# Experts of a fused attention, mixture-of-experts and channel-mix kernel: 256 tokens at a time with the first weights stationary

## The chip, the cores and the metric

The kernel runs on one core of one Trainium2 chip. A core has five engines with their own instruction streams: PE (TensorE, matrix products), DVE (VectorE), ACT (ScalarE), POOL (GpSimd) and SP (SyncE, here used for DMA alone). They share an on-chip memory (SBUF, 128 partitions) and eight banks that receive TensorE's results (PSUM, 128 partitions by 512 floats each). The metric is the device time of one execution in microseconds (us), the median of several runs. A profiled execution gives besides a trace of every instruction.

## The reference, cut to what matters

Three layers follow one another on 1536 tokens (2 sequences of 768) of width D = 512: a decayed linear attention, a mixture of 8 experts of which each token takes one, and a channel mix. The change concerns the second.

```python
for s in range(S):                      # per sequence
    fresh_e = int(np.argmax(logits[b, s]))
    if s == 0 or local_gate[b, s] < 0.5:
        e = fresh_e
    else:
        e = prev_e if prev_e >= 0 else fresh_e
    prev_e = e
    ...                                 # p: softmax of the token's logits
    h = np.maximum(x[b, s] @ w1[e], 0.0)        # w1[e]: 512 x 1024
    out[b, s] = p[e] * (h @ w2[e])              # w2[e]: 1024 x 512
```

## The kernel before

**Attention stage.** Twelve chunks of 128 tokens are computed in a software pipeline; each ends as x (128 tokens by 512), which is stored to `x_dram`, and as 9 logits a token.

**Dispatch.** From the logits each token's expert, and its place among the expert's tokens, are worked out on DVE with a few small products on PE: `rank`, `row` (place modulo 128) and `col` (expert and tile). Twelve one-hot matrices `slot_row` (POOL, L408) and twelve `slot_col` (DVE, L758) are multiplied on PE (L1017) into `slots`: for each tile of each expert the token numbers of its 128 rows. `plan` holds, for each expert, where its tiles start: an expert has as many tiles of 128 as its tokens fill, but at least `MIN_TILES = 2`. POOL gathers the rows of x for a tile by an indirect DMA (L433, L417) and scatters the result (L427).

**Experts.** For each expert a loop over its tiles. `tile` of the PE program (L1057) does: `h_products`, x times w1, with the tile's transposed x (128 columns) as the stationary operand and 512 columns of w1 moving, so that h comes out with tokens on partitions; ACT applies the ReLU into `h_sb` (L500); `h_transposes` (L1048) turns h on PE by blocks of 128x128 into `psT`; ACT copies that to `hh` (L505); `y_products` takes hh as the stationary operand and 512 columns of w2 moving; DVE copies y out of PSUM (L805). The next tile's x is transposed on PE in between (L1034).

**Three products.** Precision is held by splitting each float operand in two parts, high and low: ACT rounds a copy to the reduced format (`hh`, `xh`, `wh`), DVE subtracts it from the original (`hl` L784, `xl` L780, `wl` L790), and `three_products` multiplies high by high, high by low and low by high: three matmuls for each block (L1024 to L1026), each with its own weight load.

**Weights.** An expert's weights are 8 chunks (`CH`) of 128x1024: 4 of w1, 4 of w2. SP loads a chunk into `raw` (one buffer for the 8) when DVE has split the former content (`part_l`), two experts ahead; ACT and DVE split into one of two sets of `parts`, used by turns. This conversion for the next expert lies inside the first tile of an expert on both engines (`tile(i, e, p)`). PE waits at an expert's start for all eight chunks.

**Order.** It is written out by hand, engine by engine, with semaphores between them. `keep_warm` (L918) is idle work of PE on the identity matrix.

**After the experts.** The results come back from `y_dram` into `keep`, are weighted, transposed (L1104) and mixed; the channel mix runs in four blocks of 384 tokens. There w_k's 128x128 blocks are the stationary operand, and 384 columns of transposed tokens move.

## Time and profile before

| | us |
|---|---|
| median of 3 runs | 489.41 (488.84 to 490.62) |
| the profiled execution, its own time | 488.76 |
| its span from the first to the last instruction | 486.9 |
| PE busy | 459.2 |
| DVE busy | 260.4 |
| ACT busy | 210.9 |
| POOL busy | 92.6 |
| chunks of expert weights loaded in the loop (512 KB each) | 64 |

The time of a run contains some 2 us around the span. A matmul's duration runs from its start until its result has been written; several are under way at once, so what one costs on PE is the distance between the starts of two, not its duration. PEld is the weight load of a matmul, which the trace shows apart. A line number is that of the code above; a buffer's number is left out of its name (`bank` is any of the eight PSUM banks).

### The profile page before, as it was taken

The page shows a single profiled execution, that of the slowest core. Times are in us where ns is not written, and L with a number is a line of the kernel's source. Part 1 is how long each engine was busy: PE and PEld are TensorE (multiplying, and loading weights), DVE is VectorE, ACT ScalarE, POOL GpSimd, SP SyncE. Part 2 cuts the span into 40 slices and gives each one's busy share as a digit, 9 for nine tenths or more (in the row PEclk, how much of TensorE's full clock was granted, in tenths as well). Part 3 has the DMA queues.
Part 4 walks back from the last instruction along what each step waited for, and adds up shares of the span by engine and source line. Part 5 has one row for each costly group of instructions (what it writes and reads, how often), then busy time and mean ns, then how long its engine had stood idle before and what let it go on. Part 6 is the DMA issues. An engine that isn't in the chain of part 4 may idle for free.

```text
span 486.9 us, 7685 instructions
## 1 busy us (share of the span) xinstructions
PE 459.2 (94%) x2635; PEld 391.4 (80%) x2636; DVE 260.4 (53%) x421; ACT 210.9 (43%) x337; POOL 92.6 (19%) x137
## 2 busy tenths in 40 slices
PE   7899997699999999999999996599999999999997
PEld 7788886577878787878788884498899889889985
DVE  2677885355564737473829194495444544616401
ACT  1133331073645545464636373487244533714400
POOL 2436752522221222222222221000000000000000
PEclk9899999799999999999999999599999999999999
DMA  6999881048392929393867500700010000010001
GB/s 218 406 398 329 327 313 66 22 139 299 113 311 99 309 96 296 115 284 144 261 256 239 192 29 27 268 1 0 22 46 0 22 22 22 0 43 22 0 23 43
DMA packets 28460, 70.87 MB, mean 146 GB/s; under 512 B 3154, under 2 KB 4178, under 8 KB 28436
## 3 DMA queue, kind: packets, MB, share of 16 engines
q1 hardware_dynamic: 22946, 57.95, 33.8%
q0 software_dynamic: 2800, 9.18, 5.7%
q10 hardware_dynamic: 2690, 3.44, 2.0%
q8 instruction: 14, 0.23, 0.2%
q14 instruction: 10, 0.08, 0.1%
HBM read 59.53 MB, written 11.02 MB: 145 GB/s over the span
## 4 chain that ended last, share of the span: by engine, by line
PE 80%; DVE 9%; issue 3%; DMA 3%; POOL 2%; DVEq 1%; ACT 0%; SPq 0%; POOLq 0%; ACTq 0%
PE bank L1024 21%; PE bank L1026 20%; PE bank L1025 20%; DVE wl L790 5%; PE bank L954 3%; PE bank L943 2%; PE bank L930 2%; PE bank L964 2%; PE bank L1048 2%; PE bank L972 2%; PE bank L1034 2%; POOL slot_row L408 1%; PE bank L918 1%; PE bank L979 1%; DVE hl L784 1%
## 5 line engine op out<-in xcount | busy, mean ns | idle before, releaser
L790 DVE TENSOR_TENSOR wl<-raw,wh 128x1024 fp32r<-128x1024 f32 x64 | 74.6, 1218 | 0.0
L509 ACT ACTIVATE wh<-raw 128x1024 fp32r<-128x1024 f32 x64 | 64.1, 1054 | 0.0
L784 DVE TENSOR_TENSOR hl<-bank,hh 128x512 fp32r<-128x512 f32 x32 | 22.1, 690 | 64.0 <-ACT hh L505 64.0
L1024 PE MATMUL bank<-wh,hh 128*128 128x512 f32 x128 | 52.8, 412 | 2.6 <-DVE hl L784 1.6
L1024 PE MATMUL bank<-wh,xh 128*128 128x512 f32 x128 | 51.4, 402 | 1.7 <-DVE xl L780 1.7
L1026 PE MATMUL bank<-wh,hl 128*128 128x512 f32 x128 | 50.2, 392 | 0.0
L1026 PE MATMUL bank<-wh,xl 128*128 128x512 f32 x128 | 50.0, 391 | 0.0
L1025 PE MATMUL bank<-wl,hh 128*128 128x512 f32 x128 | 49.8, 389 | 0.0
L1025 PE MATMUL bank<-wl,xh 128*128 128x512 f32 x128 | 49.8, 389 | 0.0
L500 ACT ACTIVATE h_sb<-bank 128x512 f32<-128x512 f32 x32 | 19.1, 596 | 64.8 <-PE bank L1026 64.8
L1024 PE MATMUL bank<-xkh,wh 128*128 128x384 f32 x128 | 43.0, 336 | 0.3 <-DVE xkl L856 0.3
L1026 PE MATMUL bank<-xkh,wl 128*128 128x384 f32 x128 | 42.8, 334 | 0.0
L1025 PE MATMUL bank<-xkl,wh 128*128 128x384 f32 x128 | 42.8, 334 | 0.0
L1024 PE MATMUL bank<-wh,kkh 128*128 128x512 f32 x96 | 37.4, 389 | 0.0
L1025 PE MATMUL bank<-wl,kkh 128*128 128x512 f32 x96 | 37.4, 389 | 0.0
L1026 PE MATMUL bank<-wh,kkl 128*128 128x512 f32 x96 | 37.4, 389 | 0.0
L1024 PEld LDWEIGHTS bank<-wh,hh 128*128 128x128 f32 x128 | 24.0, 188 | 12.9 <-issue 9.1
L864 DVE TENSOR_TENSOR kk<-kk 128x384 f32<-128x384 f32 x32 | 17.7, 557 | 31.2 <-ACT kk L587 31.2
L505 ACT ACTIVATE hh<-bank 128x512 fp32r<-128x512 f32 x32 | 19.1, 597 | 29.7 <-PE bank L1048 29.7
L874 DVE TENSOR_TENSOR o_sb<-bank,r_sb 128x512 f32<-128x512 f32 x12 | 8.3, 690 | 41.6 <-PE bank L1026 41.6
L587 ACT ACTIVATE kk<-bank 128x384 f32<-128x384 f32 x32 | 15.5, 490 | 34.5 <-PE bank L1026 34.5
L1024 PEld LDWEIGHTS bank<-wh,xh 128*128 128x128 f32 x128 | 24.1, 188 | 6.2 <-issue 1.9
(159 smaller groups left out, 894.2 us busy)
## 6 DMA issues: line engine op xcount, KB each, us to landing
raw<-in_w_dram SPq DMA_DIRECT2D x64, 512.0 KB, 8.0
qk_sb<-in_qk_dram SPq DMA_DIRECT2D x12, 512.0 KB, 7.0
kv_sb<-in_kv_dram SPq DMA_DIRECT2D x12, 512.0 KB, 6.1
x_dram<-keep ACTq DMA_DIRECT2D x12, 256.0 KB, 6.2
keep<-y_dram SPq DMA_DIRECT2D x12, 256.0 KB, 5.3
out_dram<-o_sb SPq DMA_DIRECT2D x12, 256.0 KB, 2.0
raw<-in_w_k_dram SPq DMA_DIRECT2D x4, 512.0 KB
raw<-in_w_v_dram SPq DMA_DIRECT2D x4, 512.0 KB
```

The lines of the kernel that those rows point to most:

```text
L500: act.activation(h_sb[:, g * D:(g + 1) * D], bank[g][:, :], ACT.Relu).then_inc(s["h_done"], 1)
L505: act.activation(hh[:, 4 * g:4 * g + 4, :], by(psT[g][:, :], 4), ACT.Copy).then_inc(s["hh_done"], 1)
L509: act.activation(parts[1 - p][0][:, c, :], raw[:, c, :], ACT.Copy).then_inc(s["part_h"], 1)
L587: act.activation(kk[f % KK], bank[f % 4][:, 0:HB], ACT.Relu).then_inc(s["relu_done"], 1)
L784: dve.tensor_tensor(hl[:, 4 * g:4 * g + 4, :], by(psT[g][:, :], 4), hh[:, 4 * g:4 * g + 4, :].bitcast(F32), ALU.subtract).then_inc(s["hl_d ...
L790: dve.tensor_tensor(parts[1 - p][1][:, c, :], raw[:, c, :], parts[1 - p][0][:, c, :].bitcast(F32), ALU.subtract).then_inc(s["part_l"], 1)
L864: dve.tensor_tensor(kk[f % KK], kk[f % KK], kk[f % KK], ALU.mult).then_inc(s["kk_done"], 1)
L930: mm = pe.matmul(psS[t % 2][a][:, pair * P:(pair + 1) * P], lhsT=kT[r, pair, :], rhs=qT[r, pair, :], start=True, stop=True)
L954: mm = pe.matmul(psO[DH * a:DH * (a + 1), pair * P:(pair + 1) * P], lhsT=kv_sb[t % RING][:, 1, h * DH:(h + 1) * DH], rhs=AT[t % 2][:, a, p ...
L1024: pe.matmul(ps, lhsT=a_high, rhs=b_high, start=start, stop=False)
L1025: pe.matmul(ps, lhsT=a_high, rhs=b_low, start=False, stop=False)
L1026: return pe.matmul(ps, lhsT=a_low, rhs=b_high, start=False, stop=stop)
```

## The change

The unit of work of an expert becomes 256 tokens (`PAIR`), two gathered tiles side by side. The first product is turned round: 128 columns of w1 are the stationary operand and the 256 tokens of the unit move, so h comes out transposed, with the hidden dimension on partitions, four PSUM banks with two blocks of 128x256 each. ACT applies the ReLU straight from PSUM into `hh`, DVE makes `hl` from the same bank, and `h_sb` with its transposes is gone. The second product is as before, once for each half of the unit. An expert has at least one unit. The 8 chunks of weights are split in two groups: the first six are converted before the unit, the last two (`CH_LATE`) behind it, and PE waits for the first six ahead of the first product and for all eight ahead of the second. In the dispatch, DVE makes the one-hot matrices in two operations of each kind (128x576 and 128x768) instead of twelve, POOL multiplies one of them by the token numbers, and a short chain on DVE works out the column of `slots` with which each unit starts (`unit_col`).

```diff
-    MIN_TILES = 2
-    NTILES_MAX = N // P + MIN_TILES * E
+    PAIR = 2 * P
+    UNITS_MAX = N // PAIR + E
+    CH_LATE = 2
     CH = KD + KF // 2
     FIRST = 1
+    PARTS = FIRST + CH_LATE
...
 @block.gpsimd
-            pool.wait_ge(s["row_done"], 1)
-            for n in range(NT):
-                pool.tensor_scalar(slot_row[:, n, :], iota_row[:, :], row[:, n:n + 1], None, ALU.is_equal).then_inc(s["slot_row_done"], 1)
+            pool.wait_ge(s["value_done"], 1)
+            for b in range(B):
+                pool.wait_ge(s["col_hit_done"], b + 1)
+                pool.tensor_tensor(slot_col[:, b * NC:(b + 1) * NC, :], col_hit[:, b * NC:(b + 1) * NC, :], per_token(value, b),
+                                   ALU.mult).then_inc(s["slot_col_done"], 1)
+            def fetch(rows):
+                for a in range(2):
+                    pool.indirect_dma_start(out=x_tok[a], out_offset=None, in_=x_dram[:, :],
+                                            in_offset=bass.IndirectOffsetOnAxis(ap=rows[:, a:a + 1], axis=0)).then_inc(x_in[a], 16)
...
+                pool.wait_ge(s["x_ps_done"], u * 2 + 2)
+                pool.tensor_copy(x_slots[:, :], slots[:, bass.ds(next_c, 2)]).then_inc(s["x_slots_done"], 1)
...
+                fetch(x_slots)
+                for a in range(2):
+                    pool.wait_ge(s["y_done"], u * 2 + FIRST + a + 1)
...
+                    pool.indirect_dma_start(out=y_dram[:, :], out_offset=bass.IndirectOffsetOnAxis(ap=y_slots[:, a:a + 1], axis=0),
+                                            in_=y_sb[a], in_offset=None).then_inc(y_out[a], 16)
...
 @block.scalar
-            def relu_h(i, g):
-                act.wait_ge(s["h_ps"], i * 2 + g + 1)
-                act.activation(h_sb[:, g * D:(g + 1) * D], bank[g][:, :], ACT.Relu).then_inc(s["h_done"], 1)
+            def h_high(u, f):
+                act.wait_ge(s["h_ps"], u * 4 + f + 1)
+                act.activation(hh[:, 2 * f:2 * f + 2, :], by(psH[f][:, :], 2), ACT.Relu).then_inc(s["hh_done"], 1)
+            def unit(u):
+                for f in range(4):
+                    h_high(u, f)
+                for a in range(2):
+                    x_high(u + 1, a)
...
-                    tile(lo, e, p)
+                    act.wait_ge(s["raw_in"], (e + 1) * (16 * (CH - CH_LATE)))
+                    act.sem_inc(s["act_passed"], 1)
+                    for c in range(CH - CH_LATE):
+                        if c == KD:
+                            act.wait_ge(s["y_ps"], lo * 2 + FIRST)
+                            act.sem_inc(s["act_passed"], 1)
+                        weights_high(p, c)
...
+                    with act.Fori(lo, hi) as u:
+                        unit(u)
+                    act.wait_ge(s["raw_late"], (e + 1) * (16 * CH_LATE))
+                    act.sem_inc(s["act_passed"], 1)
+                    for c in range(CH - CH_LATE, CH):
+                        weights_high(p, c)
...
 @block.vector
-            for n in range(NT):
-                dve.tensor_scalar(slot_col[:, n, :], iota_row[:, 0:COLS], col[:, n:n + 1], value[:, n:n + 1],
-                                  ALU.is_equal, ALU.mult).then_inc(s["slot_col_done"], 1)
+            for b in range(B):
+                dve.tensor_tensor(col_hit[:, b * NC:(b + 1) * NC, :], iota_row[:, 0:COLS].unsqueeze(1).to_broadcast([P, NC, COLS]),
+                                  col[:, b * NC:(b + 1) * NC].unsqueeze(2).to_broadcast([P, NC, COLS]), ALU.is_equal).then_inc(s["col_hit_done"], 1)
+                dve.tensor_tensor(slot_row[:, b * NC:(b + 1) * NC, :], iota_row[:, :].unsqueeze(1).to_broadcast([P, NC, P]),
+                                  row[:, b * NC:(b + 1) * NC].unsqueeze(2).to_broadcast([P, NC, P]), ALU.is_equal).then_inc(s["slot_row_done"], 1)
...
+            def h_low(u, f):
+                dve.wait_ge(s["hh_done"], u * 4 + f + 1)
+                dve.scalar_tensor_tensor(out=hl[:, 2 * f:2 * f + 2, :], in0=by(psH[f][:, :], 2), scalar=0.0,
+                                         in1=hh[:, 2 * f:2 * f + 2, :].bitcast(F32), op0=ALU.max, op1=ALU.subtract).then_inc(s["hl_done"], 1)
+            def y_copy(u, a):
+                dve.wait_ge(s["y_ps"], u * 2 + FIRST + a + 1)
+                dve.wait_ge(y_out[a], u * 16 + 16)
+                dve.tensor_copy(y_sb[a], psY[a][:, :]).then_inc(s["y_done"], 1)
+            def unit(u):
+                for f in range(4):
+                    h_low(u, f)
+                y_copy(u, 0)
+                for a in range(2):
+                    x_low(u + 1, a)
+                y_copy(u, 1)
...
-                    tile(lo, ep * UNROLL + j, p)
+                    for c in range(CH - CH_LATE):
+                        weights_low(e, p, c)
...
+                    with dve.Fori(lo, hi) as u:
+                        unit(u)
+                    for c in range(CH - CH_LATE, CH):
+                        weights_low(e, p, c)
...
 @block.tensor
-            def h_transposes(i, g):
...
+            def h_products(p, f):
+                for i in range(2):
+                    cols = slice((2 * f + i) * P, (2 * f + i + 1) * P)
+                    for c in range(KD):
+                        mm = three_products(psH[f][:, i * PAIR:(i + 1) * PAIR], [w[:, c, cols] for w in w1p[p]],
+                                            [x[:, c, :] for x in (xh, xl)], start=(c == 0), stop=(c == KD - 1))
+                mm.then_inc(s["h_ps"], 1)
+            def y_products(u, p, a):
+                for f in range(KF):
+                    if a == 0 and f % 2 == 0:
+                        pe.wait_ge(s["hl_done"], u * 4 + f // 2 + 1)
+                    mm = three_products(psY[a][:, :], [x[:, f, a * P:(a + 1) * P] for x in (hh, hl)], [w[:, f, :] for w in w2p[p]],
+                                        start=(f == 0), stop=(f == KF - 1))
+                mm.then_inc(s["y_ps"], 1)
+            def unit(u, e, p):
+                pe.wait_ge(s["xl_done"], u * 2 + 2)
+                for f in range(4):
+                    h_products(p, f)
+                pe.wait_ge(s["part_l"], e * CH + PARTS)
+                pe.wait_ge(s["y_done"], u * 2 + FIRST)
+                y_products(u, p, 0)
+                x_unit_transposes(u + 1)
+                y_products(u, p, 1)
...
-                    pe.wait_ge(s["part_l"], FIRST + e * CH)
+                    pe.wait_ge(s["part_l"], e * CH + PARTS - CH_LATE)
```

What this does to the order of instructions on PE, in an expert's work: this is a tile of before, from the last products of the first three quarters of h to the first products of y. `wh_49` and `wl_50` are the high and low parts of the weights, the last figure is rows by moving columns, and rows of one product that repeat are left out.

```order
L1026 MATMUL bank<-wh_49,xl 128x512
L1046 REGISTER_ALU
L1048 MATMUL bank<-ident,h_sb 128x128 x4
L1024 MATMUL bank<-wh_49,xh 128x512
...
L1024 MATMUL bank<-wh_49,hh 128x512
L1025 MATMUL bank<-wl_50,hh 128x512
...
L1046 REGISTER_ALU
L1048 MATMUL bank<-ident,h_sb 128x128 x4
L1030 ISA
L1034 MATMUL bank<-ident,x_tok 128x128 x4
L1024 MATMUL bank<-wh_49,hh 128x512
```

And this is a unit of the changed kernel, from the end of h to the second half of y, on the same engine; its products of h are 96 with 256 columns where two tiles of before had 48 with 512.

```order
L1038 MATMUL bank<-xh,wl_50 128x256
L1071 REGISTER_ALU
L1072 REGISTER_ALU
L1062 ISA
L1036 MATMUL bank<-wh_49,hh 128x512
L1037 MATMUL bank<-wl_50,hh 128x512
...
L1043 ISA
L1045 REGISTER_ALU
L1047 MATMUL bank<-ident,x_tok_79 128x128 x4
L1047 MATMUL bank<-ident,x_tok_80 128x128 x4
L1036 MATMUL bank<-wh_49,hh 128x512
```

The transposes of `h_sb` are gone, and those of x for the next unit stand together between the two halves of y.

On DVE an expert of before begins with the split of its first h, and the conversion of the next expert's weights (`wl`) lies between the steps of the first tile:

```order
L784 TENSOR_TENSOR hl<-bank,hh 128x512
L789 ISA
L790 TENSOR_TENSOR wl_52<-raw,wh_51 128x1024
...
L784 TENSOR_TENSOR hl<-bank,hh 128x512
L779 REGISTER_ALU
L780 TENSOR_TENSOR xl<-bank,xh 128x512
...
L804 ISA
L805 COPY y_sb<-bank 128x512
```

In the changed kernel the copy of the second half of y is followed by the two late chunks of one set and the six early ones of the other (each row of `wl_50` stands for one of six), and only then by the split of h:

```order
L799 COPY y_sb_82<-bank 128x512
...
L804 TENSOR_TENSOR wl_52<-raw,wh_51 128x1024
L803 REGISTER_ALU
L804 TENSOR_TENSOR wl_52<-raw,wh_51 128x1024
L803 ISA
L804 TENSOR_TENSOR wl_50<-raw,wh_49 128x1024
...
L830 ISA
L793 SCALAR_TENSOR_TENSOR hl<-bank,hh 128x512
```

So eight conversions in a row now stand between a unit's last copy and the next unit's first `hl`.

## Rows read from the trace of the kernel before

**Rows 1.** The page, shares of the chain that ended last, by engine.

```profile
PE 80%; DVE 9%; issue 3%; DMA 3%; POOL 2%; DVEq 1%; ACT 0%; SPq 0%; POOLq 0%; ACTq 0%
```

**Rows 2.** Groups by form: count, busy us, mean ns, idle before and its releaser.

```profile
L784 DVE TENSOR_TENSOR hl<-bank,hh 128x512 fp32r<-128x512 f32 x32 | 22.1, 690 | 64.0 <-ACT hh L505 64.0
...
L943 PE MATMUL bank<-kv_sb,kdec 128*128 128x128 f32 x80 | 12.3, 300 | 2.7 <-POOL kdec L384 2.7
...
L851 DVE SCALAR_TENSOR_TENSOR mix<-yT,mu_sb,mix 128x384 f32<-128x384 f32 x4 | 2.4, 617 | 0.2 <-ACT mix L574 0.2
...
L384 POOL TENSOR_TENSOR kdec<-kv_sb,decay 128x512 f32<-128x512 f32 x10 | 13.3, 1338 | 12.9 <-DMA decay<-powers_dram 9.5 <-PE bank L943 3.4
```

**Rows 3.** Timeline of PE in one tile: start, duration in us, instruction.

```profile
202.38 0.39 PE L1026 MATMUL bank<-wh,xl 128*128 128x512 f32 x1
...
203.28 0.39 PE L1025 MATMUL bank<-wl,xh 128*128 128x512 f32 x1
...
204.19 0.40 PE L1026 MATMUL bank<-wh,xl 128*128 128x512 f32 x1
204.71 0.47 PE L1024 MATMUL bank<-wh,hh 128*128 128x512 f32 x1
205.02 0.39 PE L1025 MATMUL bank<-wl,hh 128*128 128x512 f32 x1
...
205.94 0.39 PE L1026 MATMUL bank<-wh,hl 128*128 128x512 f32 x1
...
207.28 0.39 PE L1025 MATMUL bank<-wl,hh 128*128 128x512 f32 x1
```

**Rows 4.** Timeline of PE: 12 distances at 512 columns, 12 at 384 columns.

```profile
146.21 0.39 PE L1026 MATMUL bank<-wh,hl 128*128 128x512 f32 x1
...
148.93 0.39 PE L1026 MATMUL bank<-wh,xl 128*128 128x512 f32 x1
...
404.84 0.33 PE L1025 MATMUL bank<-xkl,wh 128*128 128x384 f32 x1
...
406.92 0.33 PE L1025 MATMUL bank<-xkl,wh 128*128 128x384 f32 x1
```

**Rows 5.** Timeline of PE: eight loads of 128 columns and eight float products.

```profile
45.88 0.97 PEld L943 LDWEIGHTS bank<-kv_sb,kdec 128*128 128x128 f32 x8
45.88 1.16 PE L943 MATMUL bank<-kv_sb,kdec 128*128 128x128 f32 x8
```

**Rows 6.** Timeline of DVE and ACT in an expert's first tile.

```profile
160.73 0.69 DVE L805 COPY y_sb<-bank 128x512 f32<-128x512 f32 x1 [0.47 <-PE bank L1026]
161.34 4.62 DVE L790 TENSOR_TENSOR wl<-raw,wh 128x1024 fp32r<-128x1024 f32 x4
...
157.09 4.84 ACT L509 ACTIVATE wh<-raw 128x1024 fp32r<-128x1024 f32 x5
```

**Rows 7.** The page, DMA issues: KB each, median us to landing.

```profile
raw<-in_w_dram SPq DMA_DIRECT2D x64, 512.0 KB, 8.0
```

**Rows 8.** Timeline of the dispatch, to the first expert's first product.

```profile
82.26 0.17 DVE L752 SCALAR_TENSOR_TENSOR row<-over,rank 128x12 f32<-128x12 int32 x1
...
82.54 7.03 POOL L408 TENSOR_SCALAR slot_row<-iota_row,row 128x128 f16<-128x128 f16 x12 [11.66 <-DVE row L752]
...
91.14 1.08 POOL L433 DMA_INDIRECT x_tok<-x_dram,slots  x1 [1.58 <-DVE plan L767]
...
96.91 0.49 PE L1024 MATMUL bank<-wh,xh 128*128 128x512 f32 x1 [1.68 <-DVE xl L780]
```

**Rows 9.** Busy time of the engines in stretches; PEclk is the granted clock.

```profile
90.00:92.00 2.00, 2.00 (x11) 2.00 (x10) 1.76 (x10) 0.00 (x0) 0.85 (x1) 0.50 0.00 0
...
94.00:96.00 2.00, 1.24 (x12) 0.94 (x9) 0.00 (x0) 0.60 (x1) 0.30 (x2) 1.00 0.01 2
```

**Rows 10.** Timeline of the experts' end, to the first transposes behind it.

```profile
299.76 0.39 PE L1026 MATMUL bank<-wh,hl 128*128 128x512 f32 x1
...
300.29 0.69 DVE L805 COPY y_sb<-bank 128x512 f32<-128x512 f32 x1 [2.71 <-PE bank L1026]
...
308.63 2.05 PE L1104 MATMUL bank<-ident,keep 128*128 128x128 f32 x8 [8.47 <-DVE keep L839]
```

More of the change, by code:

```diff
@@ L221, in plan_of, with all_units @@
         def plan_of(eng, e):
-            lo = eng.value_load(plan[0:1, bass.ds(e, 1)], min_val=0, max_val=NTILES_MAX)
-            hi = eng.value_load(plan[0:1, bass.ds(e + 1, 1)], min_val=MIN_TILES, max_val=NTILES_MAX)
+            lo = eng.value_load(plan[0:1, bass.ds(e, 1)], min_val=0, max_val=UNITS_MAX - 1)
+            hi = eng.value_load(plan[0:1, bass.ds(e + 1, 1)], min_val=1, max_val=UNITS_MAX)
             return lo, hi
         def plan_ahead(eng, e):
-            return eng.value_load(plan[0:1, bass.ds(e + 2, 1)], min_val=MIN_TILES, max_val=NTILES_MAX)
-        def column(c, e):
-            return nc.s_assert_within(c, e * NT, e * NT + NT - 1, skip_runtime_bounds_check_because="an expert has no more tiles than all tokens fill")
+            return eng.value_load(plan[0:1, bass.ds(e + 2, 1)], min_val=1, max_val=UNITS_MAX)
+        def all_units(eng):
+            return eng.value_load(plan[0:1, E:E + 1], min_val=E, max_val=UNITS_MAX)
         def yT_at(n):
@@ L438, in _, with per_token @@
-            for e in range(E):
-                if e == 0:
-                    lo, hi = plan_of(pool, 0)
-                else:
-                    lo, hi = hi, plan_ahead(pool, e - 1)
-                with pool.Fori(lo + 1, hi) as i:
-                    gather(i, column(i - lo + e * NT, e))
-                    scatter(i - 2)
-                gather(hi, min(e + 1, E - 1) * NT)
-                scatter(hi - 2)
-            scatter(hi - 1)
-            pool.wait_ge(s["x_in"], hi * 16 + 16)
-            pool.wait_ge(s["tile_slots_done"], hi + 2)
+            def per_token(x, b):
+                return x[:, b * NC:(b + 1) * NC].unsqueeze(2).to_broadcast([P, NC, COLS])
@@ L452, in _ @@
+            for a in range(2):
+                pool.wait_ge(x_in[a], total * 16 + 16)
         @block.scalar
@@ L530, in _ @@
             act.wait_ge(s["exp_done"], 1)
+            act.wait_ge(s["x_stored"], 16 * NT)
+            for a in range(2):
+                x_high(0, a)
             act.wait_ge(s["plan_done"], 1)
-            act.wait_ge(s["mx_ps"], 1)
-            act.activation(xh, by(psX[:, :], KD), ACT.Copy).then_inc(s["xh_done"], 1)
             with act.Fori(0, E // UNROLL) as ep:
@@ L769, in _ @@
+            dve.tensor_copy(plan[:, :], tcum[:, :])
+            dve.tensor_scalar(unit_col[:, :], unit_e[:, :], 2.0, float(COLS - 2), ALU.mult, ALU.min).then_inc(s["plan_done"], 1)
             dve.wait_ge(s["exp_done"], 1)
@@ L912, in _ @@
         def _(pe):
+            pe.sem_inc(s["y_ps"], FIRST)
             pe.wait_ge(s["ident_done"], 1)
```

260 lines of the change are left out of this document (98 added, 162 removed).

## The prediction

> **What bounds the kernel now.** I read first the chain that ended last: four fifths of it lie on PE [rows 1], so what PE issues, and what it stands still for, is the time. In the expert stage the timeline gives the price of a product as the distance of two starts: 0.227 us at 512 columns (2.72 us for 12), and 0.173 us at 384 (2.08 for 12) [rows 4]; the 512 rows span the border between two tiles, which costs nothing extra. There are 32 splits of h [rows 2], two a tile, so 16 tiles: exactly the least number, 8 experts by 2, so no expert has more than 256 tokens. The stage runs from 96.91 [rows 8] to 299.76 + 0.227 = 299.99 [rows 10], 203.1 us. Its 16 x 48 = 768 products by 0.227 make 174.3; 28.8 us remain. One tile shows where they go [rows 3]: from 202.38 to 207.28 there are 14 distances between products, 3.18 us by the price, and 4.90 passed, so 1.72 a tile and 27.5 in all; 1.3 stays without a name. Of the 1.72, the first break (202.38 to 203.28, two distances) is 0.45: four transposes of h. The second (204.19 to 205.02) is 0.38: PE waits for the first `hl`. The third (205.94 to 207.28) is 0.89: four transposes of h and four of x.
>
> **The change on PE.** With at most 256 tokens an expert, the 16 tiles become 8 units.
>
> Removed: the 8 transposes of h a tile and the wait for the first `hl`. Kept: y, 48 products of 512 columns a unit, and 8 transposes of x in one place, which I price like the eight of the third break, 0.89. Changed: 48 products of h at 512 columns in two tiles become 96 at 256. The columns streamed are the same, the weight loads double. No row shows 256 columns in the reduced format. The two prices in rows 4 differ by 53 ns for 128 columns, so 256 should take 0.173 - 0.053 = 0.120. The doubt is whether the load fits beneath it. Eight loads of 128 columns of floats take 0.97 us, at most 0.121 each, and eight float products issued with them 1.16 with the last one's own 0.300, so (1.16 - 0.30) / 7 = 0.123 apart [rows 2, 5]: a load and a product of this length side by side at 0.123. I take 0.122. Bounds: below, the pure stream, 2 x 53 = 0.107; above, load and product one behind the other, 0.121 + 0.120 = 0.241. The rows of 512 columns speak against the upper end, since a load of 0.12 besides a stream of 4 x 53 = 213 ns would be 0.33, not 0.227.
>
> The Trainium skill, "TensorE: Matmul & The Clock Gate", section "LDWEIGHTS (loading the stationary operand)", gives columns / 1.2 ns for a load, so 107 ns as an estimate; the loads in rows 5 agree roughly. By it the load would hide under 0.120 with 13 ns to spare, and the sum would be 1.5 us lower than mine.
>
> A unit is then 96 x 0.122 + 48 x 0.227 + 0.89 = 11.71 + 10.90 + 0.89 = 23.50 us; eight are 188.0, with the unnamed 1.3 kept 189.3. Against 203.1 that is 13.8 us less.
>
> **What must stay hidden: DVE.** The two conversions behind the unit and the six ahead of the next now stand in one row in front of the first `hl`. Count from the unit's first product on PE. The copy of the former y starts at 0.30 (300.29 against 299.99 [rows 10]) and hands on after 0.61 (160.73 to 161.34 [rows 6]): 0.91. Eight conversions at 4.62 / 4 = 1.155 [rows 6] end at 10.15. The split of h is a new form for 512 elements from PSUM: 0.69 like the old one [rows 2], or up to 0.82, in the proportion of the 617 ns that such a three-input form takes for 384 elements [rows 2]. So `hl` is there at 10.85 to 11.0, and PE asks for it at 11.71: hidden by 0.7 to 0.9 us. The later three follow 0.7 apart and PE needs them 1.4 apart, the last at 11.71 + 18 x 0.227 = 15.8, when h itself ended 4 us earlier. If the cover goes, every microsecond costs up to 8. The copy waits only for PE. **ACT** has x high after 11.7 + 5.45 + 0.9 and two copies, some 19.5, then two late chunks and four early at 4.84 / 5 = 0.97 [rows 6] until 25.3, which is 1.8 into the next unit, two more (released at the unit's start) until 3.7; h's first quarter is ready at 2.9, so it is copied 0.8 late, and DVE is not there before 10.15 anyway. **Loads**: the sixth chunk of `raw` is free at 10.15, lands 8.0 later [rows 7] at 18.2, and ACT asks at 21.5; the late ones have a whole unit. SP's queue holds nothing else. **POOL** gathers both tiles a unit ahead, each at 1.08 [rows 8], and has 17 us for it; behind its wait for y stand only the scatter and the next gathers. All of these I cost at nothing.
>
> **Head.** Before, POOL's twelve `slot_row` take from 82.54 to 89.57 and the gather is issued at 91.14 [rows 8]. After: two small steps on DVE to 82.8, then four operations. By 690 ns for 512 elements [rows 2] the ones of 576 take 0.78 and those of 768 1.0: the second `col_hit` ends at 85.4, the second `slot_row` at 86.4, POOL's second multiplication of 576 (1338 ns for 512, rows of the same engine [rows 2]) 1.5 later, at 86.9. That is 2.6 earlier than 89.57. Then two gathers stand in a row instead of one, 1.08 to 1.9 later, and the path from the last gather's issue to the first product (91.14 to 96.91 [rows 8]) stays. The longer plan chain on DVE, 8 small steps of some 0.2, lies beside the gathers. Net 0.7 to 1.5; I take 1.0. A risk: in 90 to 92 PE was granted 0.50, its level of 1.2 GHz, after the thin stretch of slot products, and 1.00 (2.4 GHz) again in 94 to 96 [rows 9]. PE will stand longer between the two gathers; should the first products of h fall to 1.2 GHz for 3 to 4 us, it costs about 1.7.
>
> **Tail.** From the last product to 308.63 [rows 10] the chain is copy, scatter, load, weighting, and all of it stays; two late conversions slip in on DVE behind the copy, 2.3 us in a stretch in which it idles 8.5. Nothing.
>
> **Sum.** 488.76 for the profiled execution, less 13.8, less 1.0: 474.0. The median lies 0.65 above that execution, so 474.6, and I say 474.5.
>
> **Rivals.**
> Forecast, 470 to 479: 0.58.
> *The load leaves no trace* and 256 columns cost 0.107 to 0.115: 768 x (0.122 - 0.111) = 8.4 less, about 466. For it: the streams alone; against: 13 ns besides the stream at both lengths in rows 4. 0.08.
> *256 columns are dearer*, 0.13 to 0.14, since the load is as long as the product and any stagger shows: 6 to 14 more, 481 to 488. Its neighbour is the 0.123 of rows 5, which says little for it. 0.14.
> *DVE becomes the bound.* The row of eight conversions is late by 1 us beyond its cover (its steps collide with POOL's copies and gathers, or the new split is slow): 8 more, 482; no change at 1.9 us late. For it the small cover, against it that nothing of DVE's row waits for anybody. 0.10.
> *The other side: the load is not hidden under a short product.* Break-even is 14.8 / 768 = 19 ns more, a price of 0.141; at 0.241 it is 768 x 0.119 = 91 slower, 566. Place: every product of h, gaps on PE with no waiter named. Against it stand rows 4 and 5. 0.05 for all beyond 0.143. The Trainium skill, same page, section "The mechanism" (under "What overlaps and what doesn't"), says that a load overlaps running matmuls only where the row groups differ, which here they never do; by that rule this rival would hold. The 0.227 us of 512 columns disagrees with it.
> That an expert takes a second unit, so that the change would not do what it says, is excluded by the 16 tiles. The rest, 0.05, I give to waits that I do not see, with half of it slower than before.
>
> **Numbers.** About 0.5%, 2.4 us, is what this kernel's runs can tell from no change. Slower by more: 0.05 + 0.02 of the unseen + 0.01 of DVE, 0.08. Within: the upper end of dearer columns and of DVE, 0.06. Faster: 0.86. The range from 467 to 484 leaves out about half of the cheap rival (0.05) and what is beyond 484 (0.14).
>
> **What would show it.** In the changed trace: starts of h's products 0.12 apart; a unit every 23.5 us; one break of 0.9 in it; no idle of PE ahead of the first `hh` product (DVE's first split of h ends about 0.8 before it); the gather some 2.7 earlier and the first product 1 earlier. Wrong it would be by a distance above 0.13, or by `hl` arriving after h has ended.

## The result, and the profile after

The changed kernel takes 475.15 us (median of 4 runs, 472.91 to 481.17), the kernel before 490.01 (median of 4 runs); the ratio is 0.9688, with a 95% interval of 0.9652 to 0.9724. The run of 481.17, in a slower state (a mean granted clock of 0.957 against 0.971 to 0.978), is not in the ratio; the median of the other three is 474.28. The profiled execution took 472.91, with a span of 471.2. The forecast was 474.5, with 467 to 484.

The page of the changed kernel: busy time, then the shares of the chain that ended last (before in [rows 1]).

```profile
PE 443.1 (94%) x2895; PEld 399.4 (85%) x2896; DVE 262.9 (56%) x421; ACT 193.5 (41%) x306; POOL 98.5 (21%) x102
...
PE 89%; DMA 4%; DVE 2%; issue 2%; POOL 1%; ACT 1%; SPq 0%; POOLq 0%; DVEq 0%; ACTq 0%
```

PE bounds it more than before, and is as full as before (94%), in a span that is 15.8 us shorter (486.95 to 471.15). What answers to [rows 3, 4] is one unit on PE in the timeline, from the first product of its h to the first of the next unit's:

```profile
191.00 0.28 PE L1036 MATMUL bank<-xh,wh 128*128 128x256 f32 x1
...
202.52 0.40 PE L1036 MATMUL bank<-wh,hh 128*128 128x512 f32 x1
...
207.76 0.40 PE L1038 MATMUL bank<-wh,hl 128*128 128x512 f32 x1
207.99 1.04 PE L1047 MATMUL bank<-ident,x_tok 128*128 128x128 f32 x8
208.78 0.48 PE L1036 MATMUL bank<-wh,hh 128*128 128x512 f32 x1
209.10 0.39 PE L1037 MATMUL bank<-wl,hh 128*128 128x512 f32 x1
...
214.34 0.28 PE L1036 MATMUL bank<-xh,wh 128*128 128x256 f32 x1
```

The timeline shows four things. The 96 products of h take 202.52 - 191.00 = 11.52, 0.120 each. The first product of y follows without a gap. The break for x takes 209.10 - 207.76 - 2 x 0.227 = 0.89. The unit takes 23.34, and eight make the whole stage: 97.60 to 284.10 + 0.227 = 284.33, 186.7 us.

The same unit on DVE (before in [rows 6]):

```profile
191.81 9.16 DVE L804 TENSOR_TENSOR wl<-raw,wh 128x1024 fp32r<-128x1024 f32 x8
200.89 1.88 DVE L793 SCALAR_TENSOR_TENSOR hl<-bank,hh 128x512 fp32r<-128x512 f32 x3
203.35 0.69 DVE L793 SCALAR_TENSOR_TENSOR hl<-bank,hh 128x512 fp32r<-128x512 f32 x1 [0.58 <-ACT hh L502]
```

The eight conversions end 10.0 after the unit's first product, the first `hl` is done at about 201.6, and PE takes it up at 202.52. The head of the stage, in the order of time (before in [rows 8]):

```profile
82.03 0.17 DVE L748 SCALAR_TENSOR_TENSOR row<-over,rank 128x12 f32<-128x12 int32 x1
...
83.08 0.95 DVE L757 TENSOR_TENSOR slot_row<-iota_row,row 128x768 f16<-128x768 f16 x1
83.30 1.73 POOL L420 TENSOR_TENSOR slot_col<-col_hit,value 128x576 f16<-128x576 f16 x1 [13.27 <-DVE col_hit L755]
83.94 1.70 DVE L755 TENSOR_TENSOR col_hit<-iota_row,col 128x576 f16<-128x576 f16 x1
...
85.72 1.80 POOL L420 TENSOR_TENSOR slot_col<-col_hit,value 128x576 f16<-128x576 f16 x1 [0.69 <-DVE col_hit L755]
...
89.54 1.07 POOL L425 DMA_INDIRECT x_tok<-x_dram,slots  x1 [2.02 <-DVE slots L760]
...
90.92 0.97 POOL L425 DMA_INDIRECT x_tok<-x_dram,slots  x1 [0.31 <-issue]
...
95.82 0.69 DVE L788 TENSOR_TENSOR xl<-bank,xh 128x512 fp32r<-128x512 f32 x1 [0.23 <-ACT xh L497]
...
97.60 0.38 PE L1036 MATMUL bank<-xh,wh 128*128 128x256 f32 x1 [2.45 <-issue]
```

The first gather is issued 1.6 earlier than before, the second one at almost the same time as the only one of before, and the first product starts 0.69 later, 1.1 behind the end of the last `xl`, with "issue" as the only releaser. The attention stage ahead of it ended 0.2 earlier in this execution (`row` at 82.03 against 82.26), so from `row` to the first product the head is 0.9 longer: 15.57 against 14.65. The tail (before in [rows 10]):

```profile
284.52 0.69 DVE L799 COPY y_sb<-bank 128x512 f32<-128x512 f32 x1 [3.99 <-PE bank L1038]
285.13 2.35 DVE L804 TENSOR_TENSOR wl<-raw,wh 128x1024 fp32r<-128x1024 f32 x2
285.39 1.00 POOL L445 COPY y_slots<-slots 128x1 uint32 x1 [4.17 <-DVE y_sb L799]
287.28 1.06 POOL L449 DMA_INDIRECT y_dram<-y_sb,y_slots  x1 [0.90 <-POOL y_slots L445]
```

The first transposes behind the stage start at 293.57, 9.24 after the end of the last product, where it was 8.64.

So the 15.8 us of the span are, by the unrounded marks: stage 203.1 to 186.7, -16.4; up to the first product +0.7; tail +0.6; the last stage 178.3 to 177.6, -0.7.

### The profile page after: what moved, and what is told of

It is laid out like the page before. It is cut to its first block, busy times and chain, and to the rows that moved or that the text cites. A ratio compares the mean times of both kernels' runs of the same rounds, so it can differ in the third digit from the quotient of the medians.

```text
span 471.2 us, 8138 instructions
## 1 busy us (share of the span) xinstructions
PE 443.1 (94%) x2895; PEld 399.4 (85%) x2896; DVE 262.9 (56%) x421; ACT 193.5 (41%) x306; POOL 98.5 (21%) x102
## 3 DMA queue, kind: packets, MB, share of 16 engines
q0 software_dynamic: 2816, 9.18, 5.3%
## 4 chain that ended last, share of the span: by engine, by line
PE 89%; DMA 4%; DVE 2%; issue 2%; POOL 1%; ACT 1%; SPq 0%; POOLq 0%; DVEq 0%; ACTq 0%
PE bank L1036 25%; PE bank L1038 24%; PE bank L1037 24%; PE bank L965 3%; PE bank L954 3%; PE bank L941 2%; PE bank L975 2%; PE bank L983 2%; PE bank L1047 2%; PE bank L990 1%; DMA decay<-powers_dram 1%; DMA keep<-y_dram 1%; DMA x_tok<-x_dram,slots 1%; POOL slot_col L420 1%; DMA powers_dram<-pw 1%
## 5 line engine op out<-in xcount | busy, mean ns | idle before, releaser
L1036 PE MATMUL bank<-xh,wh 128*128 128x256 f32 x256 | 72.5, 283 | 2.4 <-issue 2.4
L1038 PE MATMUL bank<-xh,wl 128*128 128x256 f32 x256 | 72.4, 283 | 0.0
L1037 PE MATMUL bank<-xl,wh 128*128 128x256 f32 x256 | 72.4, 283 | 0.0
L506 ACT ACTIVATE wh<-raw 128x1024 fp32r<-128x1024 f32 x64 | 61.7, 1052 | 2.2 <-issue 1.5
L1036 PEld LDWEIGHTS bank<-xh,wh 128*128 128x128 f32 x256 | 49.1, 192 | 3.0 <-issue 2.7
L1037 PEld LDWEIGHTS bank<-xl,wh 128*128 128x128 f32 x256 | 49.1, 192 | 0.3
L1038 PEld LDWEIGHTS bank<-xh,wl 128*128 128x128 f32 x256 | 49.1, 192 | 0.0
L799 DVE COPY y_sb<-bank 128x512 f32<-128x512 f32 x16 | 11.1, 692 | 65.9 <-PE bank L1038 65.9
L497 ACT ACTIVATE xh<-bank 128x512 fp32r<-128x512 f32 x18 | 9.9, 595 | 58.9 <-PE bank L1047 58.9
L445 POOL COPY y_slots<-slots 128x1 uint32 x16 | 9.4, 590 | 109.8 <-DVE y_sb L799 109.8
```

The source lines that it names most:

```text
L497: act.activation(xh[:, :, a * P:(a + 1) * P], by(psT[a][:, :], KD), ACT.Copy).then_inc(s["xh_done"], 1)
L506: act.activation(parts[1 - p][0][:, c, :], raw[:, c, :], ACT.Copy).then_inc(s["part_h"], 1)
L799: dve.tensor_copy(y_sb[a], psY[a][:, :]).then_inc(s["y_done"], 1)
L1036: pe.matmul(ps, lhsT=a_high, rhs=b_high, start=start, stop=False)
L1037: pe.matmul(ps, lhsT=a_high, rhs=b_low, start=False, stop=False)
L1038: return pe.matmul(ps, lhsT=a_low, rhs=b_high, start=False, stop=stop)
```

## The experiments

The times of the profiled executions are read from each trace in the same four marks: DVE's `row`, the first product of h, the end of the last product of y (its start + 0.227), and the first transposes of `keep`. The head is the time from `row` to the first product.

| kernel | first product | head | stage | tail | span |
|---|---|---|---|---|---|
| before | 96.91 | 14.7 | 203.1 | 8.64 | 486.9 |
| changed | 97.60 | 15.6 | 186.7 | 9.24 | 471.2 |
| changed, second profile | 98.61 | 15.5 | 188.0 | 9.19 | 474.1 |
| before, no transposes of h | 97.52 | 14.9 | 193.2 | 8.60 | 477.9 |
| before, products of h halved | 96.93 | 14.7 | 206.0 | 8.58 | 491.6 |
| changed, 128 columns | 97.72 | 15.5 | 311.4 | 9.25 | 596.5 |
| changed, DVE + 2.3 us | 97.76 | 15.5 | 197.2 | 9.33 | 481.7 |
| changed, DVE + 0.7 us | 98.63 | 15.5 | 186.7 | 9.20 | 473.9 |
| changed, no late chunks | 97.73 | 15.6 | 187.7 | 8.58 | 472.2 |
| PE's loop written out | 99.69 | 14.5 | 189.4 | 9.28 | 477.2 |
| loop written out, no late chunks | 96.95 | 14.4 | 189.1 | 8.64 | 473.2 |
| row numbers copied early | 100.90 | 15.5 | 188.2 | 7.98 | 476.4 |
| loop written out, PE kept busy | 99.77 | 14.3 | 186.7 | 9.18 | 473.7 |
| row numbers early, loop written out, PE busy | 99.23 | 14.4 | 186.7 | 8.10 | 471.8 |

The head varies by 0.2 us or less between profiles of one code, the first product by 3.3 us. So nearly all of that scatter lies ahead of `row`, in the attention stage that the change does not touch. There the granted clock differs, from 78 to 85 us for example, in the changed kernel and in the one with the loop written out and PE kept busy:

```profile
78.00:85.00 7.00, 3.73 (x31) 2.86 (x29) 5.30 (x16) 0.14 (x1) 1.70 (x1) 1.00 0.09 36
...
78.00:85.00 7.00, 5.92 (x29) 5.33 (x30) 3.18 (x16) 0.81 (x2) 0.00 (x0) 0.53 0.20 75
```

(The columns are those of [rows 9], the granted clock third from the end.) `row` came at 82.03 in the one and at 85.44 in the other. Over the 35 runs of the kernel before that accompany the experiments, a mean granted clock lower by 0.01 goes with a time longer by 2.3 us (correlation 0.89), so medians of a few runs can differ by 1 to 2 us from this alone.

**The kernel before without the transposes of h.**

```diff
             def h_transposes(i, g):
                 pe.wait_ge(s["h_done"], FIRST + i * 2 + g + 1)
-                for f in range(4):
-                    mm = pe.transpose(psT[g][:, f * P:(f + 1) * P], h_sb[:, (4 * g + f) * P:(4 * g + f + 1) * P], ident[:, :])
-                mm.then_inc(s["hT_ps"], 1)
+                pe.sem_inc(s["hT_ps"], 1)
```

> The kernel before, with the eight transposes of h a tile left out: the second product then reads PSUM content that no transpose has written, so this part of the output is not computed. If the gain of the change comes from the transposes of h and the wait for the first hl that hangs on them, as the prediction has it, a tile loses 0.45 + 0.38 + half of 0.89, about 1.28 us, and 16 tiles some 20: 469 us. If it comes from elsewhere (fewer tile borders, the dispatch), only the array time of 128 transposes goes, under 14 us, and the wait ahead of the first hh product stays.

Measured: 479.87 us, ratio 0.9785 (0.9738 to 0.9832), half of what I expected. The stage is 9.9 shorter. That is the 14.3 at which the prediction priced the transposes, less 4.4, for the wait did not go with them: it grew. This is the second tile of an expert, on DVE and PE:

```profile
110.38 4.62 DVE L790 TENSOR_TENSOR wl<-raw,wh 128x1024 fp32r<-128x1024 f32 x4
...
114.92 0.69 DVE L784 TENSOR_TENSOR hl<-bank,hh 128x512 fp32r<-128x512 f32 x1
...
115.75 0.47 PE L1024 MATMUL bank<-wh,hh 128*128 128x512 f32 x1 [0.67 <-DVE hl L784]
```

The h was rounded at 113.72, but DVE was in its row of four conversions until 115.0. In first tiles ACT's conversions stand in front instead: `hh` starts right behind a `wh`, and DVE had been idle.

```profile
101.06 1.05 ACT L509 ACTIVATE wh<-raw 128x1024 fp32r<-128x1024 f32 x1
102.01 0.59 ACT L505 ACTIVATE hh<-bank 128x512 fp32r<-128x512 f32 x1
...
102.63 0.69 DVE L784 TENSOR_TENSOR hl<-bank,hh 128x512 fp32r<-128x512 f32 x1 [5.24 <-ACT hh L505]
```

The distance to the first `hh` product is 1.06 in second tiles and 0.61 in first ones, where 0.227 would be no wait: with 0.08 behind each, 0.69 a tile on average, 11 us in all. Before it was 0.60 and 0.52, so 0.41 a tile. So taking the transposes away is about 10 of the change's 16 us; the other 6 come from the unit of 256, whose longer h gives DVE time for its conversions (11 us of waits gone) at the price of dearer products (5 us). This split is a sum of the two kernels' stages; no run has the unit of 256 and the transposes together.

**The kernel before with halved products.** The halves of a bank were computed one after the other, so that each accumulation was closed before the next began.

```diff
-                for c in ks:
-                    mm = three_products(bank[g][:, :], [x[:, c, :] for x in (xh, xl)],
-                                        [w[:, c, g * D:(g + 1) * D] for w in w1p[p]], start=(c == 0), stop=(c == KD - 1))
+                for q in ((0, 1) if len(ks) == KD else (ks[0] // 2,)):
+                    for c in range(KD):
+                        mm = three_products(bank[g][:, q * 256:(q + 1) * 256], [x[:, c, :] for x in (xh, xl)],
+                                            [w[:, c, g * D + q * 256:g * D + (q + 1) * 256] for w in w1p[p]],
+                                            start=(c == 0), stop=(c == KD - 1))
```

> The kernel before, with each product of h of 512 columns split into two of 256, so 384 products more and as many weight loads more. By the price seen in the changed kernel (0.120 us at 256 columns against 0.227 at 512) it is 768 x 0.120 - 384 x 0.227 = 5 us slower, 494.5. If a load of its own were not hidden under 256 columns when the tokens are stationary, 0.24 each, it would be some 97 us slower; if a product cost the stream alone, no change.

Measured: 493.68 us, ratio 1.0076 (1.005 to 1.0103), 3.8 us slower, and the stage 2.9 longer. Its products of h stand 0.120 apart, which makes 5.0 more, and some 2 us come back at the breaks: the distance to the first `hh` product is 0.36 in every tile instead of 0.56 on average, 0.11 of it the shorter last product. The result excludes both other outcomes of the expectation: no change, and an unhidden load.

**The changed kernel with 128 columns.**

```diff
                 for i in range(2):
                     cols = slice((2 * f + i) * P, (2 * f + i + 1) * P)
-                    for c in range(KD):
-                        mm = three_products(psH[f][:, i * PAIR:(i + 1) * PAIR], [w[:, c, cols] for w in w1p[p]],
-                                            [x[:, c, :] for x in (xh, xl)], start=(c == 0), stop=(c == KD - 1))
+                    for q in range(2):
+                        for c in range(KD):
+                            mm = three_products(psH[f][:, i * PAIR + q * P:i * PAIR + (q + 1) * P], [w[:, c, cols] for w in w1p[p]],
+                                                [x[:, c, q * P:(q + 1) * P] for x in (xh, xl)], start=(c == 0), stop=(c == KD - 1))
```

> The changed kernel, with each product of h of 256 columns split into two of 128 (1536 instead of 768). Theory: load and product overlap, so the distance falls to the length of a load, 0.107 to 0.12, and no further: 1536 x 0.112 - 768 x 0.120 = 80 us slower, near 555. Rival one: load and product lie one behind the other at this length, 0.17 and more: 170 slower. Rival two: the stream alone counts, 0.067: 11 us slower.

Measured: 598.22 us in one run, 123 more than the changed kernel. The price itself is as the theory says; 12 distances of products in the timeline at the full clock take 1.34, so 0.112:

```profile
190.13 0.28 PE L1038 MATMUL bank<-xh,wl 128*128 128x128 f32 x1
...
191.47 0.28 PE L1038 MATMUL bank<-xh,wl 128*128 128x128 f32 x1
```

A unit at that clock takes 33.3, and eight are 266.4, 79.7 longer than in the changed kernel. Of the other 45 us, 41.7 are clock, in the first unit (54.26) and the fifth (54.07), and 3.3 a wait for `wl` at the fifth expert's start. Busy time by stretch (PE, PEld, DVE, ACT, POOL, then the granted clock):

```profile
170.00:240.00 70.00, 70.00 (x529) 65.97 (x528) 28.86 (x32) 22.11 (x28) 14.73 (x14) 1.00 0.41 151
...
280.00:300.00 20.00, 20.00 (x89) 19.27 (x90) 1.38 (x2) 1.20 (x2) 0.00 (x0) 0.53 0.00 1
```

From 97.7 to 138.7 and from 255.2 to 296.2 PE issued these products without a pause and was granted 1.2 GHz, 0.213 apart. Both stretches began behind a standstill (the head, and 3.2 us at the fifth expert's start), and 1.00 came back 3.0 and 2.5 us into the 512-column products that followed. So the distance hardly falls below 256 columns: 0.227, 0.120 and 0.112 at 512, 256 and 128, where a further 0.053 less, as between 512 and 384, would make 0.067. A product of 256 columns sits just above that floor. This fits the expectation of load and product side by side; of the clock it said nothing.

**How much DVE's row has to spare.** Two long operations, and in another kernel a short one, ahead of the first split.

```diff
             def unit(u):
+                for q in range(2):
+                    dve.tensor_reduce(mx[:, q * KD:(q + 1) * KD], xh.bitcast(F32), AX_X, ALU.max)
                 for f in range(4):
                     h_low(u, f)
```

> The changed kernel, with two more operations of DVE ahead of the first split of h in each unit (a maximum over xh, 1024 elements each, some 1.1 us, whose result nobody reads). Theory: the cover of DVE's row is 0.8 us, so seven units (the first has two conversions less in front) come 1.4 late each: 10 us slower, with PE waiting for hl ahead of its first hh product. Rival: PE does not depend on this row within a unit, no change.

Measured: 483.45 us in one run; the stage is 10.5 longer. One of seven places, DVE and PE:

```profile
155.88 2.34 DVE L809 TENSOR_REDUCE mx<-xh 128x4 f32<-128x1024 f32 x2
...
158.14 2.47 DVE L793 SCALAR_TENSOR_TENSOR hl<-bank,hh 128x512 fp32r<-128x512 f32 x4
158.87 0.19 PEld L1038 LDWEIGHTS bank<-wh,hh 128*128 128x128 f32 x1 [1.41 <-DVE hl L793]
158.87 0.50 PE L1038 MATMUL bank<-wh,hh 128*128 128x512 f32 x1 [1.21 <-DVE hl L793]
```

The first `hl` starts 12.15 behind the unit's first product where it was 9.89, so 2.26 us were added, and 10.46 / 7 = 1.49 came out a unit, 0.1 of it the slower restart of PE behind a wait. The first `hh` product itself starts 1.37 later, so some 0.9 had been spare. The changed kernel's trace says the same: its first `hl` ends 0.94 ahead of the product that needs it, and 0.05 is left where PE waits.

```diff
             def unit(u):
+                for _ in range(1):
+                    dve.tensor_reduce(mx[:, 0:KD], xh[:, :, 0:P].bitcast(F32), AX_X, ALU.max)
                 for f in range(4):
                     h_low(u, f)
```

> The changed kernel with one short operation of DVE (a maximum over 512 elements, 0.6 to 0.7 us) ahead of the first split of h in each unit. Theory: the cover measured from the other run is 2 x 1.2 - 1.2 = 1.2 us minus nothing, so 0.7 us disappear in it: no wait for hl, the stage as long as in the changed kernel, 186.7 us. Rival: PE is already at the edge of DVE's row, and every unit comes 0.5 us later, 4 us in all.

Measured: 475.69 us in one run, and a stage of 186.7 with no wait for `hl`. The first `hl` now ends 0.35 ahead of its product. The "1.2" in this expectation was worked out wrongly; the other run's figure is 0.9, and either is more than the 0.7.

**No late chunks.**

```diff
-    CH_LATE = 2
+    CH_LATE = 0
...
-                    act.wait_ge(s["raw_late"], (e + 1) * (16 * CH_LATE))
-                    act.sem_inc(s["act_passed"], 1)
```

> The changed kernel again, as the measure for the three that follow on the same chip: 474 to 475 us, ratio 0.969.

> The changed kernel with CH_LATE = 0: all eight chunks of the next expert are converted ahead of the unit, and PE waits for all eight ahead of the first product. Theory: DVE has the same eight conversions in front of the first hl, which end at the same time, and the weights are a unit ahead either way, so the stage stays at 23.3 us a unit; at the experts' end the two late conversions are gone from behind the last copy, and POOL's small copy no longer takes 1.0 instead of 0.2 us: 0.5 to 0.8 less in all. Rival: the late group is what keeps PE from waiting; then PE waits at a unit's start or for hl, by 1 us or more a unit, 8 us and more slower.

Measured on one chip: the changed kernel 475.4 us (ratio 0.9693, 0.9663 to 0.9724), this one 476.05 (0.9711, 0.9674 to 0.9748), which the runs can't tell apart. The expected gain of 0.5 to 0.8 does not show. In the trace the tail is 0.66 shorter than in the first profile of the changed kernel, as expected, POOL's copy being short again:

```profile
286.45 0.18 POOL L445 COPY y_slots<-slots 128x1 uint32 x1 [4.17 <-DVE y_sb L797]
```

But the stage is 1.0 longer, all of it in the fifth unit, which takes 24.29 instead of 23.33 because PE waits there for `hl`:

```profile
191.31 0.69 DVE L797 COPY y_sb<-bank 128x512 f32<-128x512 f32 x1 [3.98 <-PE bank L1036]
...
193.65 9.17 DVE L802 TENSOR_TENSOR wl<-raw,wh 128x1024 fp32r<-128x1024 f32 x8 [1.64 <-ACT wh L506]
...
203.48 0.50 PE L1034 MATMUL bank<-wh,hh 128*128 128x512 f32 x1 [0.69 <-DVE hl L791]
```

The first conversion follows 2.34 behind the copy's start, where it is 0.61 in the changed kernel. ACT, the releaser named, had begun its row of `wh` at 187.82 and had the first ones done, so it was not that. The fifth expert is where the program's loop over experts turns (four are written out), and DVE reads its next bounds there; in the changed kernel two late conversions lie on DVE at that place, and no gap is seen. That they hide the turn is my reading; no run isolates it, but the variant below with PE's loop written out and DVE's as it was has the same 24.29 in the same unit. So the late chunks save about 1.0 in the stage and cost 0.7 in the tail, and in the median the two come to nothing.

**PE's loop written out.**

```diff
-            keep_warm(30, psO)
-            x_unit_transposes(0)
-            pe.wait_ge(s["plan_done"], 1)
-            with pe.Fori(0, E // UNROLL) as ep:
...
+            keep_warm(20, psO)
+            pe.wait_ge(s["plan_done"], 1)
+            lo, hi = plan_of(pe, 0)
+            x_unit_transposes(0)
+            pe.wait_ge(s["first_l"], CH)
+            for e in range(E):
...
+                with pe.Fori(lo, hi) as u:
+                    unit(u, e, p)
+                if e < E - 1:
+                    hi_next = plan_ahead(pe, e)
```

> The changed kernel with PE's loop over experts written out for all eight, the first expert's bounds read ahead of the first transposes of x, and each further bound behind the unit instead of ahead of it; ten of the thirty idle products ahead of it are gone. Theory: the first product stood 1.1 us behind the last split of x because three register loads and a branch came between; it now starts 0.9 us earlier, and the rest stays: 0.9 less. Rival: something else held it (the weights, the plan), no change; or the longer code costs PE's instruction fetch at the borders, more than 1 us slower.

> Both of the former together: about 1.5 us less than the changed kernel, near 473, if they act in different places.

Measured: 475.81 us (ratio 0.9709, 0.9678 to 0.9741) and, with no late chunks besides, 476.45 (ratio 0.972, 0.9681 to 0.9759). One of the latter's six runs took 1535 us, which I can't explain; the ratio is without it, and so is a median of 475.49. The expected 0.9 and 1.5 do not show in the medians. The gap itself is gone: the first product waits for `xl` and no longer for "issue", and the head is 14.3 to 14.5 in all four profiles with the loop written out, 1.1 less than in the changed kernel. But the clock eats it. In this profile the first products stand 0.213 apart, and so they do in the second profile of the unchanged changed kernel:

```profile
98.61 0.57 PE L1036 MATMUL bank<-xh,wh 128*128 128x256 f32 x1 [2.44 <-issue]
98.98 0.41 PE L1037 MATMUL bank<-xl,wh 128*128 128x256 f32 x1
99.19 0.41 PE L1038 MATMUL bank<-xh,wl 128*128 128x256 f32 x1
```

There the stage is 1.3 us longer, here 2.7, in the first profile of the changed kernel not at all. The edit also leaves out ten of the thirty idle products ahead of the head, so a part of the longer fall may be its own doing; these profiles can't tell.

**PE kept busy, and the row numbers copied early.** On the kernel with the loop written out, idle products behind the first transposes of x; on the changed kernel, POOL's copies moved; then both.

```diff
                     mm.then_inc(s["x_ps_done"], 1)
+                    if isinstance(u, int) and u == 0:
+                        keep_warm(10 if a else 5, psO)
```

```diff
                 fetch(x_slots)
                 for a in range(2):
-                    pool.wait_ge(s["y_done"], u * 2 + FIRST + a + 1)
+                    pool.wait_ge(y_out[a], u * 16 + 16)
                     pool.tensor_copy(y_slots[:, a:a + 1], slots[:, bass.ds(c + a, 1)]).then_inc(s["y_slots_done"], 1)
-                    pool.wait_ge(s["y_slots_done"], u * 2 + a + 1)
+                pool.wait_ge(s["y_slots_done"], u * 2 + 2)
+                for a in range(2):
+                    pool.wait_ge(s["y_done"], u * 2 + FIRST + a + 1)
```

> The changed kernel, with POOL's two copies of a scatter's row numbers made right behind the gathers, not between the last copy of y and the scatter. Theory: at the experts' end the copy took 1.0 us (it met a conversion on DVE) and a wait of 0.9 came behind it; both leave the chain to the first transposes of the last stage, so the stretch of 9.2 us there shrinks to about 8.0, and the time by 1.2. Rival: the 0.9 belongs to the indirect transfer itself, and only the copy goes, 0.2 to 1.0 less; or the loads behind wait for something else, no change.

> The kernel with PE's expert loop written out, with 5 idle products behind the first tile's transposes of x and 10 behind the second's, in the 1.4 us in which PE waits for the first xl. Theory: in two of the profiles the first products of h ran at 1.2 GHz for 3 to 6 us because PE had stood nearly still before them, which costs 1.3 to 2.7 us; with PE kept busy all of the stage runs at 1.00 and the first product stays 1.4 us behind the transposes: the stage is 186.7 to 186.9 us, the median about 1 to 1.5 us below that kernel's 475.8. Rival: the clock falls by what PE did some microseconds earlier, in the thin stretch of the dispatch, and the first products are slow as often as before.

> Both of these together, on the kernel with PE's loop written out: 1.2 less by the tail and 1.5 to 2 by the head than the changed kernel, about 472.5.

Measured, on another chip than the repeat of the changed kernel: early copies 475.51 us (0.9697, 0.9665 to 0.9728), busy PE 475.23 (0.9699, 0.9671 to 0.9727), both 471.79 (0.9634, 0.9607 to 0.9661). In the traces each does its part: with early copies the tail is 7.98, 1.26 less; with idle products the clock stands at 1.00 when the stage begins, and it takes 186.7. That is two profiles of two, but of the nine of the 256-token kernel without these idle products five were granted 1.2 GHz at the stage's start or up to 1.3 us behind it and four were not, so their effect is likely, not proven. In the median each alone is hidden in the scatter ahead of `row`. Together they are faster than either alone on this chip; the interval lies below that of the changed kernel's repeat (0.9663 to 0.9724), and overlaps the first one's (from 0.9652) a little. The profile of both together, at the head:

```profile
97.16 0.66 PE L1049 MATMUL bank<-ident,x_tok 128*128 128x128 f32 x4
...
97.66 1.25 PE L931 MATMUL bank<-ident 128*128 128x128 f32 x10
...
99.23 0.39 PE L1038 MATMUL bank<-xh,wh 128*128 128x256 f32 x1 [0.32 <-DVE xl L790]
```

The idle products fill the wait for `xl`. Between this kernel and the one with busy PE alone lie 3.4 us in the median, and the tail gives 1.1 of them. The runs of this one had the higher mean granted clock, 0.978 in the median against 0.968, and by the slope above that is worth 2.3. By this estimate the rest of the 3.4 is luck of the clock; what the traces hold for is 1.1 us in the head from the loop written out and 1.1 to 1.3 in the tail from the early copies.

## Why the prediction was right

**The sum.** The forecast was 474.5, the median 475.15. From one profiled execution to the other the forecast was 14.8 less, and 15.9 was measured. That this is so near is in part luck: the stage gave 2.6 more than forecast, head (1.7) and tail (0.6) took 2.3 of it back, and the last stage, which the change does not touch, was 0.7 shorter.

**The price of 256 columns.** Taken at 0.122, measured 0.120, so the straight line through 384 and 512 columns was right and 0.123 of the float products a little high: 1.5 us of the 2.6 by which the stage came out shorter than its 189.3. The rest is about the 1.3 that I had kept as unnamed. The halved products of the kernel before gave the same order with the tokens stationary, so the price does not hang on which operand is held. At 128 columns the distance is 0.112, so a load in a row of such products costs no more than that, and the rival of loads and products in a row is refuted. So is, for this format and a whole array, the rule of the Trainium skill that loads overlap only where the row groups differ ("TensorE: Matmul & The Clock Gate", section "The mechanism", under "What overlaps and what doesn't"); the text above that rule allows a background weight buffer as well, which no run here shows or excludes. The estimate of 107 ns for a load, from the Trainium skill, same page, section "LDWEIGHTS (loading the stationary operand)", is 5% below the 0.112.

**The transposes and the wait.** The step "the 8 transposes of h a tile and the wait for the first hl" was right as a sum. But the reason that the expectation gave for the wait, that it hangs on the transposes, fell: without them it grew from 0.41 to 0.69 a tile. What it hangs on is the place of `hh` and `hl` among the conversions, on DVE in second tiles and on ACT in first ones; the unit of 256 removes it since h lasts 11.5 us and the row ends at 10.

**DVE's cover.** Forecast 0.7 to 0.9 us, measured 0.9 by overloading it, and the form of `h_low` is no dearer than the old (0.69 both). It is thin: an addition of 2.26 us a unit cost seven units 1.49 each, one of 0.6 cost nothing.

**The head.** Forecast 1.0 less, measured 0.7 more: the step that failed. Three parts of it were mis-sized. The second multiplication on POOL was to end at 86.9 and ended at 87.52: DVE's second `col_hit` took 1.70 instead of the 0.75 of the first and ended at 85.64, and the multiplication itself took 1.80 where I had 1.5. From its end to the first gather 2.02 passed instead of the 1.57 of before, because six slot products now stand behind it instead of one. The second gather followed 1.38 later, within what I had. And from the last gather to the first product it was 6.68 instead of 5.77: three register loads and a branch now stand between PE's transposes and its first product; I had carried over this path from [rows 8] as it was, though the code put a load and a loop into it. With the loop written out 1.1 of the head went, which confirms this part. The clock risk, 1.7 us by the forecast, was real: 0, 1.3 and 2.7 us in three profiles.

**The tail.** Forecast nothing, measured 0.6 more, from one collision: POOL's copy starts while DVE converts, and takes 1.0 instead of 0.18. Without the late chunks it is 0.18 again and the tail 8.58. I had named the two conversions behind the copy, and looked only at who waits for them.

## What to carry to other kernels

When a product is turned round so that its result comes out ready for the next one, count the loads: here a product of half the columns cost 0.120 against 0.227, six per cent or 5 us more for the same work, and the transposes it saved took 14; at a quarter of the columns the load is the price. Before crediting a removed operation with the wait behind it, take it out and look whether the wait is still there: it may belong to another engine's queue. When small edits are compared, measure each between marks on both sides of it in the trace, since the clock ahead of it can move the whole time by more than the edit. And if a stage starts with something read from memory (loop bounds, a plan), read it before the data arrives; idle work on PE up to the first product probably helps too.

## What the runs showed of the hardware

**Narrow products and the clock.** With 128 columns a product, PE issued products without a pause for 41 us, twice, and was granted 1.2 GHz all that time; in the other six units, entered at 2.4 GHz, it kept that through the same products. In both cases 2.4 GHz was granted again 2.5 to 3.0 us into the 512-column products that followed. In four profiles with 256 columns the clock was at 1.2 GHz at the stage's start or fell within 1.3 us of it; 2.4 GHz came back 3.1 to 6.0 us after the stage's start, still among the 256-column products.

**DVE and POOL stand in each other's way at the start of an operation.** POOL's copies of 128x1 and 128x2, 0.18 us by themselves, took 0.99 to 1.04 in all 15 cases of the changed kernel's profile in which they began inside a DVE conversion (`wl`, both inputs in SBUF), and each ended 0.04 to 0.05 behind that conversion:

```profile
192.07 1.00 POOL L445 COPY y_slots<-slots 128x1 uint32 x1 [4.17 <-DVE y_sb L799]
...
195.45 1.02 POOL L439 COPY x_slots<-slots 128x2 uint32 x1 [0.43 <-issue]
```

In the kernel before it is 0.93 in the same way, eight times. Beside an `hl` or `xl`, which read one input from PSUM, the copy kept its 0.18. DVE's `col_hit`, 0.75 by itself, took 1.70 when it began inside POOL's multiplication, ending 0.6 after it. The two `slot_row` operations, which began just before POOL's, kept their 0.95. So the later of the two waits for the earlier one to end, as far as these durations show; that both inputs in SBUF are the condition is my reading, and no experiment was made on it alone.
